# Two corner turns of an FFT convolution on TensorE instead of through DRAM, in a fused filter and mixture-of-experts kernel

## The reference

```python
X = np.fft.rfft(x, axis=1)                       # x: 8 batches x 3072 x 256, float32
y = np.fft.irfft(X * (filt_r + 1j * filt_i)[None], n=3072, axis=1)
x = y.reshape(8 * 3072, 256)                     # tokens of the layer behind it
logits = x @ w_gate                              # 256 x 8
expert = argmax(logits); gate_w = softmax(logits)[expert]
# the first 768 tokens of each expert, in token order, are kept:
h = relu(x[kept of e] @ w1[e])                   # 256 x 1024
out[kept] = gate_w * (h @ w2[e])                 # 1024 x 256; all other rows are 0
```

## Time and profile before

| | us |
|---|---|
| Median of three executions | 540.87 |
| Lowest and highest | 538.6, 543.45 |
| The profiled execution, its own time | 543.3 |
| Its span, first to last instruction | 541.3 |

### The profile page before, as it was taken

How to read it: one execution, slowest core, us unless ns; L and a number is a source line. 1 busy time by engine, 2 the same in 40 slices (tenths; PEclk the granted TensorE clock), 3 DMA queues, 4 the chain that set the end, 5 groups by cost and what they waited for, 6 DMA issues and landing times.

```text
span 541.3 us, 10327 instructions
## 1 busy us (share of the span) xinstructions
PE 460.6 (85%) x4190; PEld 368.3 (68%) x4190; DVE 246.9 (46%) x381; ACT 206.0 (38%) x362; POOL 202.3 (37%) x181
## 2 busy tenths in 40 slices
PE   5454977899789757988988998999999999998994
PEld 2112323345445424477988998999999999997994
DVE  2058235465666989578716332345412534133210
ACT  2301433455345314534135533344543436333221
POOL 0140100000000000637355788655867556684222
PEclk9958878999989977988999999999999999999998
DMA  8899897998597825999513209931099130681001
GB/s 298 298 361 413 279 380 240 316 377 275 171 339 250 281 72 151 375 409 380 192 61 106 79 11 360 377 129 40 31 332 386 54 134 30 223 316 46 30 22 44
DMA packets 63224, 117.28 MB, mean 217 GB/s; under 512 B 7632, under 2 KB 35056, under 8 KB 62656
## 3 DMA queue, kind: packets, MB, share of 16 engines
q1 hardware_dynamic: 38560, 75.77, 39.0%
q0 software_dynamic: 8864, 23.46, 12.4%
q10 hardware_dynamic: 15744, 17.31, 10.1%
HBM read 58.29 MB, written 58.23 MB: 215 GB/s over the span
## 4 chain that ended last, share of the span: by engine, by line
PE 58%; DVE 9%; DMA 5%; issue 5%; ACT 3%; SPq 2%; ACTq 0%; POOL 0%; POOLq 0%; DVEq 0%
PE psum L1335 23%; PE psum L1321 22%; PE psum L558 3%; PE psum L519 2%; PE psum L692 2%; PE psum L503 2%; DVE prod L832 2%; DMA w_raw<-in_w 2%; SPq L399 1%; PE psum L573 1%; DMA t_scratch<-t_out 1%; DVE hot_lo L983 1%; DMA g_in<-y_rows,token 1%; DMA u_scratch<-v_out 1%; PE psum L538 1%
## 5 line engine op out<-in xcount | busy, mean ns | idle before, releaser
L1146 DVE SCALAR_TENSOR_TENSOR hl<-psum,hh 128x384 fp32r<-128x384 f32 x128 | 69.0, 555 | 150.5 <-ACT hh L1098 113.5
L1335 PE MATMUL psum<-w2h,hh 128*128 128x256 f32 x384 | 109.8, 286 | 0.0
L1335 PE MATMUL psum<-w2h,hl 128*128 128x256 f32 x384 | 108.6, 283 | 0.0
L1335 PE MATMUL psum<-w2l,hh 128*128 128x256 f32 x384 | 108.6, 283 | 0.0
L832 DVE TENSOR_TENSOR prod<-psum,fab 128x1024 f32<-128x1024 f32 x48 | 56.5, 1219 | 90.8 <-PE psum L503 58.1
L1321 PE MATMUL psum<-xh,w1h 128*128 128x384 f32 x256 | 88.0, 344 | 9.6 <-DVE hl L1146 5.0
L1098 ACT ACTIVATE hh<-psum 128x384 fp32r<-128x384 f32 x128 | 60.7, 492 | 72.4 <-PE psum L1321 55.9
L1321 PE MATMUL psum<-xh,w1l 128*128 128x384 f32 x256 | 86.9, 339 | 0.0
L1321 PE MATMUL psum<-xl,w1h 128*128 128x384 f32 x256 | 86.8, 339 | 0.0
L1235 POOL DMA_INDIRECT out<-o_out,token x48 | 50.6, 1054 | 84.5 <-ACT o_out L1107 66.8
L1335 PEld LDWEIGHTS psum<-w2h,hh 128*128 128x128 f32 x384 | 73.6, 192 | 0.2 <-issue 0.2
(11 more groups left out here) (108 smaller groups left out, 536.5 us busy)
## 6 DMA issues: line engine op xcount, KB each, us to landing
out<-zero SPq DMA_DIRECT2D x24, 1024.0 KB
w_raw<-in_w SPq DMA_DIRECT2D x14, 1024.0 KB
u_scratch<-v_out ACTq DMA_DIRECT2D x48, 192.0 KB, 3.9
z_in<-t_scratch SPq DMA_DIRECT2D x24, 256.0 KB, 4.6
x_in<-in_x POOLq DMA_DIRECT2D x12, 512.0 KB, 12.3
t_scratch<-t_out SPq DMA_DIRECT2D x15, 256.0 KB, 6.3
t_scratch<-t_out ACTq DMA_DIRECT2D x15, 256.0 KB, 6.5
x_in<-in_x SPq DMA_DIRECT2D x6, 512.0 KB, 6.3
```

The source lines that it names most:

```text
L1146: nc.vector.scalar_tensor_tensor(out=hl[:, b % 2, f, :], in0=ps[(2, 3, 6, 7)[f % 4]][:, 0:TOK], scalar=0.0, in1=hh[:, b % 2, f, :].bitcast ...
L1335: mm = nc.tensor.matmul(ps[4 + (b * ST + s) % 2][:, 0:D], hx[:, b % 2, f, s * P:(s + 1) * P], wt[k][:, f, :], start=(f == 0 and m == 0), s ...
```

## The change

Both scratch tensors go. The first stage now holds the data stationary (`x_in`, 128x128) and streams `wa` (128 columns), so that its result comes out with the channels on the partitions; ScalarE writes it to `t_in`, and `pe_turn_z` transposes it to `z_in`, 64 transposes per batch in 16 banks. The way back is swapped too: `pe_inverse` holds 64x64 pieces of `prod` stationary and streams `wbi`, now 96 columns, in 32 matmuls on tiles of 64 x 64; its result lands in `v_in` with the channels on the partitions. `pe_logits` takes that directly, in front of the last transform stage, which the logits of a batch then pass in one small matmul (`pe_route_in`). `pe_turn_v` transposes `v_in` for the products, 48 transposes per batch, for the half batch as well; the transposes of y go. All the work but `pe_forward` and `pe_inverse` takes its turn in three PSUM banks (`work`), each of which ScalarE must have emptied before TensorE takes it again. `wbi` doubles to 1.5 MB, `dve_sums` works in place, the stages have a new order with eight steps each, `z_in` has four buffers, and expert 1's weights are split by VectorE within block 0 (`dve_experts`) rather than before it.

```diff
-ZB = 3
+ZB = 4
+WORK = 3
...
+STEPS_BY = [0, 2, 4, 8, 16, 24, 27, 28]
...
+def turned_at(h):
+
+    return range(6 * h, 6 * h + 6) if h < 2 else range(0)
+
+
+def products_at(t, h):
+
+    return range(4 * h - 8, 4 * h - 4) if 2 <= h < 2 + products(t) // 4 else range(0)
+
+
+def first_at(after_tokens, h):
+
+    if after_tokens:
+        return range(4 * h - 20, 4 * h - 16) if h >= 5 else range(0)
+    return range(3 * h - 12, 3 * h - 9) if h >= 4 else range(0)
...
-    zt = nc.dram_tensor("t_scratch", [NB, 2 * HR, PAIRS * D], F32).ap()
-    vt = nc.dram_tensor("u_scratch", [NB, 2, PAIRS, HR, D], F32).ap()
...
+        work = [psum[:, i].rearrange("p k d -> p (k d)") for i in range(WORK)]
+        back = [psum[:, i].rearrange("p k d -> p (k d)")[:, 0:DH * 4 * HR] for i in (3, 6)]
+        wide = psum[:, 4:6]
...
         def pe_inverse(pe, t, j):
...
-            for c in range(2):
+            for h in range(DH):
                 for a in range(2):
-                    for q in range(NQ):
-                        quarter = slice(q * QR, (q + 1) * QR)
-                        mm = nc.tensor.matmul(back[part(a), q, :], wbi[quarter, j, a, c, :],
-                                              yy[quarter, n % 2, a, c, :], start=(c == 0), stop=(c == 1))
+                    for c in range(2):
+                        for low in range(2):
+                            for q in range(2):
+                                d = h * P + low * A1
+                                at = (h * 2 + a) * 2 * HR
+                                mm = nc.tensor.matmul(back[q][part(low), at:at + 2 * HR], prod[part(q), n % 2, 0, a, c, d:d + A1],
+                                                      wbi[part(q), j, a, c, :], start=(c == 0), stop=(c == 1))
             mm.then_inc(bi_done, 1)
...
+        def pe_a(pe, t, i, first):
             c, h = divmod(i, 2)
...
-            nc.tensor.matmul(ps[i % 2][:, :], wa[:, :], x_in[:, c, 2 * h:2 * h + 2, :],
-                             start=True, stop=True).then_inc(a_done, 1)
...
+            k = next_work("pe")
+            free_work(pe, k)
+            for n in range(CH):
+                mm = nc.tensor.matmul(work[k][:, n * P:(n + 1) * P], x_in[:, c, n, h * P:(h + 1) * P], wa[:, :],
+                                      start=True, stop=True)
+            mm.then_inc(a_done, 1)
+            held[k] = (t_evac, t * 12 + i + 1)
+
+        def pe_turn_z(pe, t, g, r):
...
+            for j in range(2):
+                k = next_work("pe")
+                free_work(pe, k)
+                for i in range(2):
+                    for h in range(DH):
+                        p = GP * g + 2 * j + i
+                        mm = nc.tensor.transpose(work[k][:, (i * DH + h) * P:(i * DH + h + 1) * P],
+                                                 t_in[:, h, 2 * p:2 * p + 2].rearrange("p a r n -> p (a r n)"), ident)
...
+        def pe_logits(pe, t, s):
+            if s == 0:
+                pe.wait_ge(v_evac, 2 * NG * (t + 1))
...
+        def pe_turn_v(pe, t, i):
+            k = next_work("pe")
+            free_work(pe, k)
+            for n in range(2):
+                for h in range(DH):
+                    mm = nc.tensor.transpose(work[k][:, (n * DH + h) * P:(n * DH + h + 1) * P], v_in[:, h, 2 * i + n, :], ident)
...
+        def pe_stage(pe, t, r, a, tok, first):
+            for h in range(NG):
+                pe_forward(pe, t, r, h)
+                if tok is not None:
+                    if h == 0:
+                        if tok > first:
+                            pe_table(pe, tok - 1, 7)
+                        pe_logits(pe, tok, 0)
+                        pe_logits(pe, tok, 1)
+                    for i in turned_at(h):
+                        pe_turn_v(pe, tok, i)
+                    if h == 0:
+                        pe_raw(pe, tok)
+                    if h == 1:
+                        pe_route_in(pe, tok)
+                    if h == RANK_STEP:
+                        pe_rank(pe, tok, 7)
+                if h + ZB < NG:
+                    pe_turn_z(pe, t, h + ZB, r)
+                if h > 0:
+                    pe_inverse(pe, t, h - 1)
+                if tok is not None:
+                    for i in products_at(tok, h):
+                        pe_product(pe, tok, i)
+                if a is not None:
+                    for i in first_at(tok is not None, h):
+                        pe_a(pe, a, i, first)
+            if a is not None:
+                pe_turn_z(pe, a, 0, r)
+                pe_turn_z(pe, a, 1, r)
             pe_inverse(pe, t, NG - 1)
...
+            if a is not None:
+                pe_turn_z(pe, a, 2, r)
+                pe_turn_z(pe, a, 3, r)
...
         def pe_last(pe, t, r):
...
+            pe_table(pe, t - 1, 7)
+            pe_logits(pe, t, 0)
+            pe_logits(pe, t, 1)
+            for k, i in enumerate(half_order() if t == HALF else range(N2 // 2)):
+                pe_turn_v(pe, t, i)
+                if k == 3:
+                    pe_raw(pe, t)
+                if k == 7:
+                    pe_route_in(pe, t)
+            for i in range(products(t)):
+                pe_product(pe, t, i)
+            for k in range(WORK):
+                free_work(pe, k)
             if r == 0:
+                pe_block_turn(pe, r, 0)
...
-            nc.scalar.copy(buf[:, c % 3, 2 * h:2 * h + 2, :],
-                           ps[i % 2][:, :].rearrange("p (n d) -> p n d", d=D)).then_inc(t_evac, 1)
-            if h == 1:
-                t_store(act, t, c, 0)
+            nc.scalar.copy(t_in[:, h, :, :, c * CH:(c + 1) * CH],
+                           work[k].rearrange("p (n r u) -> p u r n", n=CH, r=2)).then_inc(t_evac, 1)
...
+            for q in range(2):
+                act.wait_ge(bi_done, t * NG + g + 1)
+                u = 16 * g + 8 * q
+                nc.scalar.copy(v_in[:, :, :, u:u + 8], back[q].rearrange("p (h x n) -> p h n x", h=DH, n=N2)).then_inc(v_evac, 1)
...
+                    if f == 1:
+                        dve.wait_ge(w_loaded[0], (r * (E - 1) + 1) * 16)
+                        nc.vector.tensor_copy(w1h[1][:, :, :].rearrange("p h f -> p (h f)"), raw_of(1, 0)).then_inc(w1h_done, 1)
+                    if f == 4:
+                        low_split(dve, r, 1, 0)
```

More of the change, by code:

```diff
@@ L377, in v_ready @@
[L377 to L399 removed]
+            return slice(a * A1, (a + 1) * A1)
@@ L593, in pe_raw @@
[L593 to L609 removed]
+                    mm = nc.tensor.matmul(ps[7][part(s), raw_at:raw_at + E * HN], wai[:, 0:A1],
+                                          lg_u[:, s * E * HN:(s + 1) * E * HN], start=True, stop=True)
+            else:
+                mm = nc.tensor.matmul(ps[7][:, raw_at:raw_at + E * N2], wai[:, :], lg_u[:, :], start=True, stop=True)
@@ new lines, in pe_route_in, with pe_product @@
+            mm.then_inc(logits_done, 1)
+        def pe_product(pe, t, i):
+            pe.wait_ge(vt_evac, t * 12 + 12 if t != HALF else t * 12 + 2 * i + 2)
+            k = next_work("pe")
+            free_work(pe, k)
+            if t == HALF:
+                for s in range(2):
+                    n = s * HN + 2 * i
+                    mm = nc.tensor.matmul(work[k][part(s), :], wai[:, 0:A1], x_in[:, n // CH, n % CH:n % CH + 2, :],
+                                          start=True, stop=True)
+            else:
+                c, h = divmod(i, 2)
+                mm = nc.tensor.matmul(work[k][:, :], wai[:, :], x_in[:, c, 2 * h:2 * h + 2, :], start=True, stop=True)
+            mm.then_inc(ya_done, 1)
+            held[k] = (ya_evac, ya_before(t) + i + 1)
@@ L695, in pe_last @@
         def pe_last(pe, t, r):
-            pe.wait_ge(v_evac, (t + 1) * NG)
-            if r == 0:
-                pe.wait_ge(p_done, 2 * (t + 1) * NG)
-                for _ in range(UNUSED):
-                    nc.tensor.matmul(ps[2][:, 0:3 * P], ident, sq[:, :, :], start=True, stop=True)
-            pe_table(pe, t - 1, 4)
-            for i in range(span(t)):
-                pe_tokens(pe, t, i, t + 1, True, t - 1)
-                if r == 0 and i == products(t):
-                    pe_block_turn(pe, r, 0)
+            pe_table(pe, t - 1, 7)
@@ L816, in act_last @@
         def act_last(act, t, r):
-            act_split(act, r, 0, 0)
+            act_logits(act, t, 0)
+            act_logits(act, t, 1)
+            for k, i in enumerate(half_order() if t == HALF else range(N2 // 2)):
+                act_turned_v(act, t, i, k)
+                if k == 3:
+                    act_raw(act, t)
+            for i in range(products(t)):
+                act_rows(act, t, i)
+            if r == 0:
+                act_block_turned(act, r, 0)
             act_split(act, r, 0, 1)
-            for i in range(span(t)):
-                act_tokens(act, t, i, True, False)
-                if r == 0 and i == products(t):
-                    act_block_turned(act, r, 0)
         def dve_multiply(dve, t, r, h):
@@ L1112, in act_experts @@
```

(20 more changed lines are left out.)

696 lines of the change are left out of this document (230 added, 466 removed).

## The result

The changed kernel takes 520.13 us (median of 4 runs, 518.55 to 521.28), the kernel before beside it 539.74 us (4 runs, 538.11 to 543.45): a ratio of 0.9625, interval 0.9564 to 0.9687. That is 3.75% less where the likeliest case said 0.9%. It lies inside the range of 519 to 560, but only 1.1 us from its lower end. The profiled execution took 519.22 us with a span of 517.4 at a mean granted clock of 0.983, against 543.3, 541.3 and 0.942.

A forecast was written before the change was run, and what follows sets the result against it. Experts bound by TensorE; the front by DMA until 110 us, then TensorE, then a chain of waits. Likeliest case: block 0 at 224, plus 307.6 and 5 given back, a 536.6 us span (538.6 in all, 536 on the median); range 519 to 560.

The forecast's parts named there:

- First stage and transposes: TensorE in the front: 0.96 us per first-stage bank, 0.44 per four transposes, load and stream overlapping.
- rival 4: Weight loads don't hide: first-stage bank 1.76 us, inverse over 2.1; 569 us in all, chance 0.06.
- The inverse: `pe_inverse` on TensorE: 1.6 us for 64 records, between bounds of 1.45 and 3.6; before it took 1.03.
- Hand-offs, 0.3 us a step: Allowance for hand-offs in front steps paced by TensorE, 0.3 us added to each step's work.
- Stage lengths: Sums of step times in the front: stage 0 44.6 us, to 69.8; stage 1 64.4 us, to 134.2.
- Stage 2 and its clock: Steps 0 to 4 by TensorE 40.2 us, then VectorE's pace 22, plus 4 for half clock: to 200.
- Tail: Last inverse to block 0: table, logits, transposes, products and splits, 21.8 us plus 2 for the clock, to 224.
- Give-back: Block 0: splitting expert 1's weights there delays the table; 5 of 5.4 us lost (0 to 6).
- rival 1: Front quicker: hand-offs hide (-5), inverse at 1.45 (-2.7), block 0 has room for the split (-4); 525 us, chance 0.22.
- rival 2: ScalarE's copies pace the three work banks, 0.1 us more on each of 120 banks: 556 us, chance 0.18.
- rival 3: Slower clock: 0.8 in stretches with waits adds an estimated 12 us to the front; 548 us, chance 0.12.
- DMA at nothing: In the front, remaining transfers need less than half of 310 GB/s and cost nothing beside TensorE's work.

The follow-up runs named there:

- inverse_twice: Changed kernel with each inverse group's 32 matmuls issued twice: 556.1 us against 540.35 for the kernel before, ratio 1.0288.
- The pair of byte experiments: Four extra DRAM-to-DRAM copies (12.6 MB) at the start of stage 1, in the changed kernel (534.17 us, 0.9881) and the kernel before (577.99 us, 1.0707).
- half_both: Kernel before with half of each corner-turn row not transferred (15.7 MB less) and fixed routing: 542.22 us, 0.9874; that routing alone 548.82 us.
- warm: Changed kernel with 36 unused matmuls in TensorE's pauses of steps 5 to 7 of the last stage: 529.09 us, ratio 0.9684.
- split_late_warm: Changed kernel with expert 1's split ahead of block 0, the y-store wait moved to the first o_out write, and 36 unused matmuls: 526.06 us, 0.967.
- two_banks: Changed kernel with two PSUM work banks instead of three: 540.63 us, ratio 0.9899 to the kernel before.
- after_bytes: Changed kernel with four extra DRAM-to-DRAM copies (12.6 MB) issued by GpSimd at the start of stage 1: 534.17 us, ratio 0.9881.
- split_early: Changed kernel with VectorE's split of expert 1's weights moved ahead of block 0: 531.17 us, ratio 0.9732.

## Why the prediction was right in kind and too small

The mechanism was the one forecast, and the size was not. The prediction gave faster than 535.5 us a chance of 0.41, slower 0.31, so its direction was a weak bet. That 520.13 is inside the range at all is a matter of 1.1 us; the 3.5 us behind the table, which nothing in the change explains, brought it that near to the end.

- *What bounds it, and what goes.* Right: TensorE-bound front, 37 MB gone for the 38 worked out, no DMA wait left, experts' arithmetic untouched. inverse_twice shows the first for stages 0 and 1. The pair of byte experiments shows that the kernel before was at the limit of its transfers, half_both that bytes are a part of the gain and not all.
- *First stage and transposes.* Right. `3.77 us` for four banks is 0.94 a bank against 0.96 taken. That is 0.118 us a record. A load of 128 columns alone is an estimated 0.11 (two records of 8 columns take 0.22), and a stream of 128 columns an estimated 0.113 (a product's eight records of 512 columns take 3.63 us). Added they would be 0.22, so load and stream overlap, and rival 4 (569 us) didn't come. By the sentence of the Trainium skill, "TensorE: Matmul & The Clock Gate", section "The mechanism", that a load overlaps only "when row_grp differs", they would add; this trace doesn't agree. It agrees with what the same section says ahead of that sentence, that a load can also go ahead into "the background weight buffer".
- *The inverse.* Taken at 1.6 from bounds of 1.45 and 3.6; measured 1.48 at full clock, in all steps on the path but the last (2.84). It goes at 23 ns a record, where 96 columns on one of four tiles would make an estimated 21 by the product's 3.63 us. Eighteen steps by 0.12 are 2.2 us.
- *Hand-offs, 0.3 us a step.* This is the step that failed most. In the stretches that TensorE binds there are none: the chain goes from 1.48 to 1.02 to 1.02 without a gap (82.55 to 86.07). Over 4 + 8 + 5 steps that is 5 us too much. The prediction gave no row for the 0.3. The trace of before does have such a gap, in front of the first product of a group (`PE psum L558 <- issue: 2.0, 8, 0.3` in the list of its waits), but the changed kernel has it no more: the gap belonged to that order of work.
- *Stage lengths.* Stage 0 measured 44.7 for 44.6, and that is luck. Its steps 0 to 3 took 16.8 us for 16, steps 4 to 7 21.7 for 23.2 (no hand-offs, a shorter inverse), and its end 6.3 for 5.4. The errors cancel. Stage 1 measured 61.6 for 64.4: hand-offs -2.4, eight inverses -1.0, logits (2.76 for 3.4) -0.6, products -0.6, first stage and small matmuls -0.4, in sum -5.0. Against that stand +2.1: the transposes take more than their 0.44 a bank (8.0 us for 7.0 and 5.8 for 5.3), and one wait for the last copy to `t_in` is 0.6.
- *Stage 2 and its clock.* 60.7 for 62.1 + 4. Steps 0 to 4 took 37.6 us for 40.2. From there to the end it is 23.1 for the 22 of VectorE's pace. The clock did fall, to 0.78 at 180 to 200 us, but it made the last inverse 1.4 us and the table behind it 0.7 us longer and little else, since VectorE was the one that TensorE waited for. 4 us for it were too many, warm gives 2.3.
- *Tail.* 20.2 for 21.8 + 2. The clock was 0.99 in 200 to 220 us; the 2 us for it weren't needed, and the logits took 0.6 us less. The tail's own terms (1.2, 3.4, 8, 5.5 and 3) add up to 21.1 and not to 21.8.
- *Give-back.* 2.3 for 5, and for another reason: that the sign is right is luck. The prediction put the split of expert 1's weights on the path. It isn't there: warm and split_late_warm reach the table in the same 34.3 and 34.2 us with and without it, so rival 1 was right that block 0 has room for it. (The cast itself fell from 3.50 to 1.22, since it no longer lies beside GpSimd's operation.) What was given back is a routing step that now stands beside that operation until it ends, 2.73 us for 0.35. No term of the prediction had it.
- *Copies.* Right: 0.586, rival 2 not met with three banks; two_banks shows how near it was. *Clock*: rival 3 (0.8 in the front) didn't come.
- *DMA at nothing.* Right for this kernel, wrong as a reason: after_bytes shows that the cover is thin.

In sum, against 536.6 and by the marks of the table: -1.3 at the start, +0.1 in stage 0, -2.8 in stage 1, -5.1 in stage 2 with its clock, -3.8 in the tail, -2.8 in the give-back and -3.5 behind the table: 19.2 us, the span of 517.4. Of the 15.7 us ahead of the table some 8 are allowances put on top of the sums (thirteen hand-offs of stages 1 and 2, 3.9 us; 4 of the 6 us for the clock), all on the same side. Rival 1 named the hand-offs, the inverse and the give-back with 12 us and got 0.22; in hindsight that was too low a chance.

## What to carry to other kernels

Where an engine binds a stretch and its inputs are on the chip, price the stretch as the bare sum of the pitches that the chain shows, and name for every allowance the row and the order of work that it comes from; several small ones, all on one side, were half of this forecast's miss of 3%. Compare stage by stage, too: a total that fits can be made of errors that cancel, and this gain of 15 us has a stage in it that got 5.5 us longer. A DMA round trip between two on-chip steps could be bought back here with TensorE work, with three PSUM banks so that ScalarE's copies run alongside, and what decided was whether small matmuls go at the pace of their streams. A cost read from a row holds for the neighbours that it had there: here a step moved away from GpSimd's large operation got cheaper, and one moved beside it dearer. And a difference between two profiles is not yet the price of the edit between them: go through both chains piece by piece first.

## What the runs showed of the hardware that was not expected

- Beside GpSimd's 4.5 us TENSOR_TENSOR of 128x2048 some operations of VectorE stand until it ends: a step of 192 elements with both inputs in SBUF took 2.73 and 3.87 us in block 0, where it takes 0.35 in stage 2, and both times ended 0.21 us behind GpSimd's operation. An operation that reads PSUM went on in its 0.56 us. How long the stand is depends on when the step starts: 1.44 us in split_early.
- 64 records on four 64x64 tiles go at 23 ns each, though each needs its own load of 64 columns and 96 of stream.
- TensorE stops of 1.9 to 4.4 us with no releaser turn up at the end of the front, in warm and inverse_twice in stretches where the DMA share is 1.01 to 1.04, and after_bytes has two in stage 1, under its copies, that the changed kernel hasn't. The changed kernel has one of 1.03 us at 39.2 us with DMA nearly idle, though. Their cause wasn't tried.
- The experts' part of one and the same kernel varied from 270.5 to 274.3 us between two executions on two chips, with 0 to 31.5 us of VectorE's idle time under "issue".
